# One part and one PSUM bank for the border counts of each routing level

## The reference, cut to what matters

```python
# first mixture: greedy by logit, each expert takes at most cap tokens
logits = x @ w_gate                       # 22784 tokens x 8 experts
for idx in np.argsort(-logits.flatten()):
    tok, e = (int(idx) // E, int(idx) % E)
    if assigned[tok] >= 0 or counts[e] >= cap:
        continue
    assigned[tok] = e
    counts[e] += 1
...
h = np.maximum(x[mask] @ w1[e], 0.0); out[mask] = h @ w2[e]
# second mixture
expert_idx = np.argmax(logits, axis=1)    # of the new logits
out[mask] = gate_w[mask, None] * ye
```

## Time and profile before

| | us |
|---|---|
| median of 3 runs | 2315.74 (2313.95 to 2320.16) |
| profiled execution, its own time | 2332.93 |
| its span, first to last instruction | 2331.1 |
| TensorE busy | 1953.3 (84%) |
| VectorE busy | 1288.8 (55%) |
| ScalarE busy | 950.9 (41%) |
| GpSimd busy | 722.1 (31%) |
| mean granted TensorE clock | 0.92 of 2.4 GHz |

### The profile page before, as it was taken

One profiled execution on the slowest core, in us unless ns is written; L12 is line 12 of the kernel. 1 busy time (PEld: TensorE's weight loads), 2 busy tenths in 40 slices (PEclk: granted clock), 3 DMA queues, 4 the chain that ended last, 5 costly groups with the idle time before them and its releaser, 6 DMA issues.

```text
span 2331.1 us, 36413 instructions
## 1 busy us (share of the span) xinstructions
PE 1953.3 (84%) x10729; PEld 1517.2 (65%) x10729; DVE 1288.8 (55%) x4137; ACT 950.9 (41%) x2046; POOL 722.1 (31%) x618
## 2 busy tenths in 40 slices
PE   7886898699723988787878787987959999999998
PEld 3343444355422766565666665765759999999998
DVE  2224777422388675656666665511246666666665
ACT  2334777422111333333333232433435555555554
POOL 0001000000054344443534454345424343444434
PEclk9898999899955999998989898988979999999999
DMA  6876999787784010101110101111168888888885
GB/s 187 263 238 217 308 308 308 205 210 205 198 304 149 17 41 27 41 24 40 28 40 27 45 26 45 39 32 31 32 226 281 283 276 287 275 283 280 280 283 175
DMA packets 161018, 382.35 MB, mean 164 GB/s; under 512 B 29813, under 2 KB 88876, under 8 KB 135581
## 3 DMA queue, kind: packets, MB, share of 16 engines
q1 hardware_dynamic: 120749, 287.59, 39.1%
q10 hardware_dynamic: 11696, 57.94, 7.2%
q0 software_dynamic: 28480, 35.66, 5.4%
HBM read 273.07 MB, written 109.13 MB: 164 GB/s over the span
## 4 chain that ended last, share of the span: by engine, by line
PE 54%; issue 16%; POOL 9%; DMA 9%; DVE 7%; SPq 2%; another core or an unknown queue 1%; ACT 1%; ACTq 0%; DVEq 0%; POOLq 0%
PE bank L951 8%; PE bank L952 8%; PE bank L953 8%; POOL sorted L1659 5%; PE bank L864 5%; DMA arena<-in_dft_mid_dram 4%; POOL xr L1650 4%; PE bank L767 3%; PE bank L768 2%; DMA arena<-in_h_dram 2%; PE bank L788 2%; PE bank L688 2%; PE bank L689 2%; PE bank L750 2%; PE bank L885 2%
## 5 line engine op out<-in xcount | busy, mean ns | idle before, releaser
L1154 ACT ACTIVATE arena<-bank 128x356 f32<-128x356 f32 x512 | 239.3, 469 | 564.9 <-PE bank L887 385.3
L864 PE MATMUL bank<-arena 128*128 128x356 f32 x1024 | 407.4, 481 | 0.0
L1553 DVE SCALAR_TENSOR_TENSOR hlo<-bank,hhi 128x374 fp32r<-128x374 f32 x544 | 297.7, 548 | 192.3 <-ACT hhi L1187 132.8
L1187 ACT ACTIVATE hhi<-bank 128x374 fp32r<-128x374 f32 x544 | 263.2, 484 | 251.7 <-PE bank L953 209.1
L1687 POOL DMA_INDIRECT out_dram<-orow,slot x204 | 247.4, 1213 | 382.0 <-DVE slot L1592 324.7
L1650 POOL DMA_INDIRECT xr<-conv_y,idx x192 | 217.5, 1133 | 217.2 <-PE bank L828 144.2
L885 PE MATMUL bank<-xhi,wsp 128*128 128x356 f32 x512 | 261.5, 511 | 14.8 <-ACT arena L1154 6.3
L1659 POOL DMA_INDIRECT sorted<-arena,slot x192 | 193.7, 1009 | 164.9 <-DVE slot L1332 102.1
L951 PE MATMUL bank<-xhi,wsp 128*128 128x374 f32 x544 | 193.4, 356 | 3.3 <-DMA wsp<-w_split 3.3
L864 PEld LDWEIGHTS bank<-arena 128*128 128x128 f32 x1024 | 188.1, 197 | 0.7
L1631 POOL TENSOR_TENSOR wsp<-arena,wsp 128x1024 fp32r<-128x1024 f32 x16 | 40.4, 2530 | 469.1 <-ACT wsp L1104 469.1
(11 more groups left out here) (216 smaller groups left out, 3730.7 us busy)
## 6 DMA issues: line engine op xcount, KB each, us to landing
wsp<-w_split SPq DMA_DIRECT2D x136, 1024.0 KB, 5.3
arena<-spec_a SPq DMA_DIRECT2D x90, 320.0 KB, 3.5
spec_a<-arena ACTq DMA_DIRECT2D x16, 1600.0 KB
spec_b<-arena SPq DMA_DIRECT2D x90, 256.0 KB, 3.5
arena<-spec_b SPq DMA_DIRECT2D x16, 1280.0 KB
arena<-in_dft_mid_dram SPq DMA_DIRECT2D x90, 192.0 KB, 4.4
arena<-in_moe_w_dram SPq DMA_DIRECT2D x32, 512.0 KB, 6.3
w_split<-wsp ACTq DMA_DIRECT2D x16, 1024.0 KB, 6.3
```

The costliest lines, as they stand in the source:

```text
L864: r = mm(bank[Z1[t % 2]][:, 0:T1], w2raw[u][:, f * D:(f + 1) * D], h32[:, f, :], start=(f == 0), stop=(f == FC - 1))
L1154: nc.scalar.activation(h32[:, f, :], bank[H1[q % len(H1)]][:, 0:T1], ACT.Relu).then_inc(m_hh[0], 1)
L1187: nc.scalar.activation(hh[:, f, 0:T], bank[f % 4][:, 0:T], ACT.Relu).then_inc(m_hh[m_], 1)
L1553: v.scalar_tensor_tensor(hl[:, f, 0:T], bank[f % 4][:, 0:T], 0.0, hh.bitcast(F32)[:, f, 0:T], ALU.max, ALU.subtract).then_inc(m_hl[m_], 1)
```

## The change

All borders of a level become one part: one signal from VectorE after the last border, 12 matmuls of 240 columns (272 in level 7) into bank 6 in place of 12 of 128 and 12 of 112 (144), one signal back, one `dcnt` and one `rcnt` over all borders. The requests of a level fall from three to two (`DREQ`). Bank 7 is used by the ranks alone until the ties; the wait for `m_pr` moves from the counts to a place ahead of `ties`.

```diff
-PARTS = (0, 8)
+PARTS = (0,)
...
-        CNT = (6, 7)
+        CNT, RANK = (6,), 7
...
-                mm(bank[CNT[1]][:, RK:RK + E * n], tri[:, :], ohb[:, 0:E * n], start=True, stop=True)
+                mm(bank[RANK][:, RK:RK + E * n], tri[:, :], ohb[:, 0:E * n], start=True, stop=True)
...
                     for part, b0, b1 in parts_of(nb):
-                        if part == 1 and j and pending(st, j - 1) is not None:
-                            pe.wait_ge(m_pr, pending(st, j - 1) + 1)
                         count(n, part, b0, b1)
...
                 moe1(due(st, at_), due(st, at_ + TIES))
+                if pending(st, NL - 2) is not None:
+                    pe.wait_ge(m_pr, pending(st, NL - 2) + 1)
                 ties(st * NREQ + NREQ - 1)
```

More of the change, by code:

```diff
@@ L850, in ranks @@
                     pe.wait_ge(li_gc, EC // 2 * E)
-                mm(bank[CNT[1]][:, RK:RK + E * n], tri[:, :], ohb[:, 0:E * n], start=True, stop=True)
-                mm(bank[CNT[1]][:, TOT:TOT + E * n], ones[:, :], ohb[:, 0:E * n].rearrange("p (k e) -> p e k", e=E),
+                mm(bank[RANK][:, RK:RK + E * n], tri[:, :], ohb[:, 0:E * n], start=True, stop=True)
+                mm(bank[RANK][:, TOT:TOT + E * n], ones[:, :], ohb[:, 0:E * n].rearrange("p (k e) -> p e k", e=E),
                    start=True, stop=True).then_inc(m_pf, 1)
@@ L1318, in gate_place @@
                 dve.wait_ge(m_pf, i + 1)
-                own.did(v.tensor_copy(added[:, :, 1:1 + n], bank[CNT[1]][:, TOT:TOT + E * n].rearrange("p (e k) -> p e k", e=E)))
+                own.did(v.tensor_copy(added[:, :, 1:1 + n], bank[RANK][:, TOT:TOT + E * n].rearrange("p (e k) -> p e k", e=E)))
                 own.then(v.tensor_scalar(gsum[:, 0:n], gsum[:, 0:n], 1e-9, None, ALU.add))
@@ L1324, in gate_place @@
                 own.wait()
-                v.tensor_tensor(per_k(rank, n), per_k(bank[CNT[1]][:, RK:], n), first[:, :, 0:n].rearrange("p e k -> p k e"),
+                v.tensor_tensor(per_k(rank, n), per_k(bank[RANK][:, RK:], n), first[:, :, 0:n].rearrange("p e k -> p k e"),
                                 ALU.add).then_inc(m_pr, 1)
```

## The result

The changed kernel takes **2291.47 us** (2288.43 to 2301.45, 6 runs) where the kernel before, run beside it, takes 2319.1 (2313.95 to 2335.73, 6 runs): 0.988 of it, with an interval of 0.9857 to 0.9904. That is 28 us faster. The forecast was 2325.3 and slower, and its range began at 2302. Its profiled execution took 2292.75 us, with a span of 2290.9; TensorE is busy for 1936.3 us of it (85%), VectorE for 1268.5.

A forecast was written before the change was run, and what follows sets the result against it. Round 0 was taken as bound by a level's chain, later rounds by TensorE's waits for VectorE. Terms 9.0 + 2.9 + 3.5 - 0.3 - 5.5 = +9.6 us on the median 2315.74 gave 2325.3 us, range 2302 to 2338.

The forecast's parts named there:

- The late signals: Levels 2 and 6, rounds 2 to 6: TensorE's signals reach VectorE late; one signal saves 5.5 us, bounds +3.5 and -19.5.
- levels 0 and 4 (+3.5): Single signal arrives when part 1's did; the wider dcnt and rcnt add 0.25 us, 14 times, +3.5 us.
- The rival of the freed signals: Each TensorE signal takes a turn while GpSimd issues, so one fewer makes all behind it earlier; 2301 us, chance 0.19.
- The bound of the same step: Late levels, rounds 2 to 6: a level 2 gives at most 2.3 to 2.5 us, a level 6 at most 1.4.
- Round 0, +9.0: Counts wait for the fifteenth border, then a wider dcnt and rcnt: 1.10 us a level, 1.35 in level 7; bounds +3, +12.
- the rival of the slack: Round 0: GpSimd's delays move under the longer count, so it costs 3 us and not 9; 2317 us, chance 0.15.
- Levels 1, 3 and 5, +0.16: Rounds 1 to 6: one part makes xcnt start 0.16 us later in 18 levels, +2.9 us.
- TensorE's own time unchanged: Counting matmuls: 12 wide ones take as long as 24 narrow ones, taken as zero change.
- Level 7, the waits, the ties: Level 7: two instruction pairs become one, -0.3 us, counted in round 1 alone; moved m_pr wait and ties cost nothing.
- the rival of the clock: Later xcnt in levels 0 and 4 adds a half-clock TensorE stretch once a round; +28 us, 2344, chance 0.12.

The follow-up runs named there:

- The runs on chip C: Changed kernel with 12 matmuls and one or two signals, or 24 and one or two, against the kernel before: 0.9874, 0.9841, 1.0047, 1.0043.
- the narrow and the wide kernel with two signals: Changed kernel plus a second signal nobody waits for, counts in 24 matmuls (narrow) or 12 (wide): 2198.55 and 2198.16 us, 1.0057 and 1.0061 of the kernel before.

## Why the prediction was wrong

**The late signals: the step that failed.** The forecast took it that a level's last signal hangs on GpSimd's run alone, gave the single signal the date of part 1's in levels 0 and 4 (+3.5) and half of its way to part 0's in level 2 (-5.5), and let the relu stay as late as it was. Its rival had the lateness go with the number of signals. The runs on chip C showed neither: it goes with the number of TensorE's load and matmul pairs while GpSimd issues indirect DMAs. Halving them brought levels 0, 4 and 6 back to 1.43 us and level 2 down by 3 us a time. Measured, levels 0 and 4 with the two of round 1 gave -9.1 (-7.3 and -1.8) and not +3.5, levels 2 and 6 of the late rounds -26.9 and not -5.5: 34 us in all below the forecast's terms. That the relu came 8.0 us after the counts in all five rounds was taken as a date set by GpSimd's run, and it was none: with half of the matmuls it comes 3.3 us earlier in four of the five rounds and 2.6 in the other. The rival of the freed signals, at 2301, foresaw a gain of the right kind from a count of signals, which is not what sets it, and fell short of it by 10 us.

**The bound of the same step.** At most 2.3 to 2.5 us for a level 2 and 1.4 for a level 6 were worked out with a relu that stays late. They gave 3.0 and 2.4. The bound, not only the value between the bounds, was wrong.

**Round 0, +9.0: mis-sized, by place.** From the first border to the last `total` it took 66.3 to 72.1 us in seven profiled executions with two parts, 69.3 on average, and 68.5 to 78.6 in eight with one wide part, 72.3: +3.0, the lower of the two bounds, though single executions of each kind spread by 2 to 3 us, so that the 3.0 is good to some 3 us either way. In a level that GpSimd leaves alone the steps are as forecast (`dcnt` 2.62 us after the counts, `total` 3.84). What falls away is the waiting for GpSimd: in levels 3 to 6 `total` came 5.1 to 5.8 us after the counts, and now 3.84. So the rival of the slack was nearer here. On chip E, too, one part and two in round 0 are 1.7 us apart, within their spread.

**Levels 1, 3 and 5, +0.16: right in levels 3 and 5.** There `total` starts 2.65 us after the counts in place of 2.48, +0.17. Level 1 gave nothing: from round 2 on it had taken 2.68 to 2.70 before. The 18 levels together gave +1.0 and not +2.9.

**TensorE's own time unchanged: right.** 1.39 us for 12 x 240 columns, 1.42 for 24 narrow ones. From start to start the matmuls are 102 to 103 ns apart at 240 columns, 55 to 56 at 128 and 49 to 50 at 112, so that twelve fewer save 0.03 us a level, and on chip A the narrow and the wide kernel with two signals are 2198.55 and 2198.16. The Trainium skill ("TensorE: Matmul & The Clock Gate", section "Back-to-back issue gap") gives 81 ns for a load and matmul pair at 128 columns. The traces do not agree with it; they show 55 to 56.

**Level 7, the waits, the ties: right.** Level 7 changed by -0.1 us over six rounds (-0.3 forecast), TensorE has no idle time ahead of the matmul of the ties in rounds 1 to 6, where the wait for `m_pr` now stands, and VectorE still waits at the ties beside the run of twelve scatters (8.68 us in round 2 against 9.49; 51.4 us over the rounds against 51.5). Nothing speaks for the rival of the clock: PEclk is 0.97 in round 1 as before, and over the whole execution 0.926 against 0.919.

Added up, the terms as measured are +3.0, +1.0, -9.1, -0.1 and -26.9, -32 us, where the medians are 28 apart.

**Not settled.** By what way GpSimd's indirect DMAs hold up TensorE's signals; whether the results are late or only the signals, since a matmul's end is modelled (the next steps' matmuls start on time behind the counts); why a chip like A or D shows none of it; why level 7 is on time beside a joined run of 21 in three rounds and held for 19 us beside a run of 9 and one of 12 in another. The changed kernel as it stands wasn't timed on a chip without late signals; its nearest kin there, the one with two parts in round 0 and the one with a second signal, are 0.3% and 0.6% slower than before.

## What to carry to other kernels

Where a consumer takes up a TensorE result some us after its matmuls, beside a gapless run of GpSimd's indirect DMAs, count TensorE's instructions, not its columns or signals: the same sums in half as many matmuls were worth 1.2 to 1.6% here, though their own time didn't change. Where such a run can be made shorter, try it, and look at every level after it: six DMAs in place of nine gave the kernel before 0.5%, and the same move cost the changed kernel 24 us at another level. Time such a change on more than one chip, since its nearest kin were slower than before where nothing was late; and if a wait has been put down to another engine's date, don't use that date as a bound until one run has moved it.

## What was not expected of the hardware

- The kernel before takes 2185 to 2193 us on two chips and 2317 to 2335 on the others, some 6% more; with the gathers on SyncE, rounds 1 to 6 take 604.7 us on chip D and 684.9 on chip E.
- TensorE's signals arrive up to 3.4 us late with 12 wide matmuls (4.84 in place of 1.43, chip C), 6.5 with 24 (8.05 in place of 1.53), 10.7 with 24 beside twelve scatters (12.22 in place of 1.53, chip E) and 17.3 with 12 (18.9 in place of 1.59, chip F). In level 3, which has no such run beside it, they are on time in every round (1.53 before, 1.43 to 1.44 after). ScalarE's relus are held with VectorE's counts.
- Twelve matmuls of one column each, 0.38 us in all, made a level 2 later by 2.9 us.
- The times of executions without a profile agree: on chip C the profiled execution of the changed kernel took 2303.67 us with a median of 2305.8 over all, so the time lost is no effect of recording.
